# Delaying GpSimd's products of the next half, and moving six weight splits, in a fused linear-attention and two-MLP kernel

## The chip, the cores and the metric

The kernel runs on one core of a Trainium2 chip. The metric is the device time of one execution in microseconds (us), lower is better. The program is written engine by engine: TensorE (matmuls), VectorE, ScalarE, GpSimd and SP (which issues all DMAs) each have a list of instructions that they run in order, and semaphores hold them together.

## The reference

Three stages follow each other: a linear attention with a decaying state, a gated MLP and an ELU MLP. All data is float32.

```python
# r, k, v, w: (B=4, H=8, S=768, D=48); u: (H, D)
for t in range(S):
    cur = einsum('bhd,bhe->bhde', u * kt, vt)
    y[:, :, t] = einsum('bhd,bhde->bhe', rt, state + cur)
    state = wt[..., None] * state + einsum('bhd,bhe->bhde', kt, vt)
x = y.transpose(0, 2, 1, 3).reshape(3072, 384)
x = (sigmoid(x @ w_gate) * (x @ w_val)) @ w_out          # d_ff = 1536
h = x @ w2_in                                            # d_ff = 2048
out = where(h > 0, h, exp(min(h, 0)) - 1) @ w2_out
```

## The kernel before

**Halves.** The sequence is cut into 6 blocks of 128 steps, and each block into two halves of 2 batches: 12 halves q = 0 to 11. Within a half the 16 (batch, head) pairs are worked as G = 8 pairs of heads, in two sub-steps b = 0 and 1 of 4 pairs each. A half is a fixed list of steps (`STAGES`): the transposes Tw, Tr, Tk of w, r and k on TensorE, the levels L1 to L6, the transposes KT of the decayed k, then Y (the output) and S (the new state).

**Levels.** The scores A[s, t] = sum over d of r_t k_s times the decays between s and t are built in levels of block length 1, 2, 4, up to 64. At each level TensorE multiplies (L597, and L603 for the last), VectorE multiplies r by a decay (`next_level_r`, L879, and L883 for the last level), GpSimd multiplies k (`next_level_k`, L513), and VectorE or ScalarE puts the level's scores into A (L922; L711).

**Near entries.** A's diagonal and the entries next to it are not made by matmuls. GpSimd's `term` makes three elementwise products per half: "r'k" (L490, r one step later times k), "rk" (L495) and "u" (L502, two instructions, one per b). VectorE sums them (`sum_after` L888, `sum_own` L892) into `dots`, selects them into `near` (L933, L935) at step L5, and at steps KT copies them into A with a predicated copy (L941), one per b. The semaphore `d_diag` counts these copies. TensorE's Y (L617) of sub-step b waits for it.

**Where the products stand.** At step KT of b = 1 GpSimd first scales the state (L531, two instructions) and then makes the three products of the half q + 1. Nothing of half q holds them; they begin as soon as GpSimd gets there. The sum of "r'k" stands on VectorE's list at step S of the same half, the sum of the others at step Tw of half q + 1.

**Dense work.** Layer 1 of the first MLP is done for sets of tokens as their halves are ready. Its thirds ("g", "v", "o" and a part i = 0 to 2; lines L657 and L666) are interleaved with the attention steps of the next halves in one list, `PROGRAM`, that all engines follow. The first 28 steps are all of half 0 and the first 4 of half 1, and then comes the split of y. float32 operands are cut into a high part (ScalarE, L711) and a low part (VectorE: xl L968, hl L972), and three of the four products are taken. After the attention the second MLP runs alone (L682, L690).

**W1's splits.** The weights of the first MLP lie in 36 pieces (12 column blocks of w_gate, w_val and w_out). Each is loaded by SP (L370, L371, L373) into one of 8 raw places, and split once: ScalarE copies the high part into `WS` and VectorE subtracts it (L993, semaphore `d_wlo`). `SPLIT1` says behind which step of `PROGRAM` each split stands: pieces 0 to 5 behind the steps L5, L6 and KT of half 0, one each, and the others behind each third part of set 0's dense groups. Piece 8 and later ones are loaded into places that an earlier piece leaves, so SP waits for `d_wlo` ahead of them. Pieces 8 to 11 stand on SP's queue just ahead of `move_y(0)` (L380), which brings the rest of half 0's output into place for the dense layer.

Of the kernel before, what the change touches and what calls it, by code (L numbers as in the profile page):

```python
# [13 lines left out]
def build(nc, r, k, v, w, u, w_gate, w_val, w_out, w2_in, w2_out, out):  # L14
# [16 lines left out]
    B, H, S, D = r.shape  # L31
# [8 lines left out]
    U = B // HALF  # L40
# [56 lines left out]
    def count(*use):  # L97

        return PLACE_OF[use] + 1
# [29 lines left out]
    PROGRAM = USES[:LEAD] + [("x", 0)]  # L129
    done = LEAD  # L130
    phase = {}
    for m in range(NS):
        room = len(THIRDS[m]) - (9 if len(SETS[m][1]) == 2 else 14)
        if m + 1 < NS:
# [4 lines left out]
            if m in MORE:  # L139
# [4 lines left out]
                PROGRAM = PROGRAM[:-len(tail)]  # L144
# [8 lines left out]
    assert done == len(USES) and len(set(PROGRAM)) == len(PROGRAM) == len(USES) + NS + sum(len(x) for x in THIRDS + LATE)  # L153

    N1 = 3 * F1
    EARLY = [("a", 0, name, b) for name in ("L5", "L6", "KT") for b in range(U)]
    AHEAD = len(EARLY)

    def splits(step):

        return step in EARLY or (step[:2] == ("d", 0) and step[-1] == 2)


    SPLIT1 = {step: x for x, step in enumerate([step for step in PROGRAM if splits(step)][:N1])}
    SPLIT2 = {("d", NS - 1, "v", j + 1, 2): j for j in range(F1 - 2)}
    assert len(SPLIT1) == N1

    DOWNS = F2 - 1 + B
    STEPS2 = []
# [9 lines left out]
    with ctx:  # L179
# [3 lines left out]
        def sem(name):  # L183
            return ctx.enter_context(nc.semaphore(name))
# [71 lines left out]
        d_w, d_dots, d_near, d_diag = sem("d_w"), sem("d_dots"), sem("d_near"), sem("d_diag")  # L256
# [3 lines left out]
        def wait(eng, s, value):  # L260

            if not (isinstance(value, int) and value <= 0):
                eng.wait_ge(s, value)
# [31 lines left out]
        def level(q, li, b, n=NL):  # L295

            return 2 * n * q + 2 * li + b + 1
# [159 lines left out]
        def _(pool):  # L457
# [50 lines left out]
            def next_level_k(q, li, b):  # L508
                L = 2 ** li
                pool.wait_ge(d_w, NL * q + max(li, 1))  # L510
                Kb = blocks(K[:, b * PR:(b + 1) * PR], L)
                Wb = decay(li)[:, b * PR:(b + 1) * PR].rearrange("q g (i two) -> q g i two", two=2).unsqueeze(4)
                gp.tensor_tensor(Kb[:, :, :, 0, :], Kb[:, :, :, 0, :],  # L513
                                 Wb[:, :, :, 1].to_broadcast([P, PR, P // (2 * L), L]), ALU.mult).then_inc(p_k, 1)

            def attention(q, name, b):
                hf = q % HALF
                if name == "Tk":
                    pool.wait_ge(a_evac, EVAC * q + 4 + b + 1)
                    next_level_k(q, 0, b)  # L520
                elif name[0] == "L":
                    li = int(name[1:])
                    pool.wait_ge(s_att, count("a", q, name, b))
                    pool.wait_ge(p_k, level(q, li - 1, b))
                    next_level_k(q, li, b)
                elif name == "KT" and b == 1:
                    wait(pool, d_s, 2 * q)

                    for e in range(2):
                        rows = slice(e * HP, (e + 1) * HP)  # L530
                        gp.tensor_tensor(SW[rows], ST[rows, hf, :, e, :], decay(NL)[rows].to_broadcast([HP, G, D]),  # L531
                                         ALU.mult).then_inc(p_sw, 1)
                        pool.wait_ge(p_sw, 2 * q + e + 1)
                    if q + 1 < NQ:
                        for part in ("r'k", "rk", "u"):
                            term(q + 1, part)
                if q == 0 and (name, b) in FIRST_TERMS:
                    term(q, FIRST_TERMS[name, b])
# [170 lines left out]
        def _(act):  # L709
            def copy(o, i):  # L710
                return nc.scalar.activation(o, i, ACT.Copy)  # L711
# [86 lines left out]
            def split_w1(x):  # L798
                act.wait_ge(w1_loaded[x], 64 if x % 3 < 2 else 16)
                copy(w1_piece(x, 0), w1_raw(x)).then_inc(a_whi, 1)  # L800
# [43 lines left out]
            for step in PROGRAM:  # L844
                if step[0] == "a":
                    attention(*step[1:])
                elif step[0] == "x":
                    split_y(step[1])
                else:
                    layer1(*step[1:])  # L850
                if step in SPLIT1:
                    split_w1(SPLIT1[step])
                if step in SPLIT2:
                    split_w2(SPLIT2[step])
                if step == ("d", NS - 1, "v", F1 - 1, 2):
                    split_x(0)
# [8 lines left out]
        def _(dve):  # L865
# [125 lines left out]
            def split_w1(x):  # L991
                dve.wait_ge(a_whi, x + 1)
                tt(w1_piece(x, 1), w1_raw(x), f32(w1_piece(x, 0)), ALU.subtract).then_inc(d_wlo, 1)  # L993
# [36 lines left out]
            for step in PROGRAM:  # L1030
                if step[0] == "a":
                    attention(*step[1:])
                elif step[0] == "x":
                    split_y(step[1])
                else:
                    layer1(*step[1:])
                if step in SPLIT1:
                    split_w1(SPLIT1[step])
                if step in SPLIT2:
                    split_w2(SPLIT2[step])  # L1040
                if step == ("d", NS - 1, "v", F1 - 1, 2):
                    split_x(0)
# [26 lines left out]
```

## Time and profile before

| | |
|---|---|
| median of 3 runs | 1128.24 us (1127.53 to 1129.59) |
| profiled execution | 1124.52 us |
| its span | 1122.8 us |
| TensorE matmul busy | 1062.5 us (95%) |
| weight load busy (beside it) | 921.1 us (82%) |
| VectorE busy | 663.4 us (59%) |
| ScalarE busy | 482.6 us (43%) |
| GpSimd busy | 268.2 us (24%) |
| mean granted TensorE clock | 0.977 |

Times in a timeline are microseconds from the start of the span. An instruction's duration includes time in which it is held by a shared resource. A number in brackets behind a row is how long the engine sat idle ahead of it, and what released it. PE is TensorE, DVE is VectorE, ACT ScalarE, POOL GpSimd, and SPq the queue of DMA issues. A granted clock of 1.00 is 2.4 GHz, 0.50 is 1.2 GHz.

### The profile page before, as it was taken

What the parts mean: (1) busy time and instruction counts of PE and PEld (TensorE: products, weight loads), DVE (VectorE), ACT (ScalarE), POOL (GpSimd) and SP (SyncE); (2) the same over time, 40 slices, a digit from 0 to 9 for tenths busy, and PEclk for the clock granted to TensorE, in tenths of its full rate; (3) what the DMA queues carried; (4) which work ended last, traced back from release to release, by engine and by line L of the source; (5) the groups of instructions that cost most, each with busy time, mean ns of one, the idle gap of its engine ahead of it and who ended that gap; (6) DMA issues with size and microseconds to landing.
All of it is one profiled execution on the core that took longest, in us unless ns stands there. A gap on an engine that the chain in (4) does not pass through costs nothing.

```text
span 1122.8 us, 19998 instructions
## 1 busy us (share of the span) xinstructions
PE 1062.5 (95%) x8124; PEld 921.1 (82%) x8124; DVE 663.4 (59%) x914; ACT 482.6 (43%) x895; POOL 268.2 (24%) x258
## 2 busy tenths in 40 slices
PE   4677789999999999999999999999999999999998
PEld 4576778878787888888787888799899999999998
DVE  6878687787948785876678433353434333343433
ACT  2535433534343344334343333464445454454543
POOL 8424162444615351624253100000000000000000
PEclk7699999999999999999999999999999999999999
DMA  7573504041213404050500051120101010010000
GB/s 142 81 134 86 96 2 68 20 65 31 39 46 51 67 2 81 17 68 5 92 5 1 5 155 57 46 82 1 57 2 57 1 43 14 1 57 1 29 1 29
DMA packets 146651, 51.44 MB, mean 46 GB/s; under 512 B 116352, under 2 KB 144256, under 8 KB 146560
## 3 DMA queue, kind: packets, MB, share of 16 engines
q1 hardware_dynamic: 146560, 50.16, 22.4%
q8 instruction: 65, 1.06, 0.4%
q14 instruction: 26, 0.21, 0.1%
HBM read 39.52 MB, written 9.44 MB: 44 GB/s over the span
## 4 chain that ended last, share of the span: by engine, by line
PE 85%; DVE 8%; issue 2%; ACT 2%; SPq 1%; DMA 1%; POOL 0%; DVEq 0%; POOLq 0%; ACTq 0%
PE ps L657 26%; PE ps L690 18%; PE ps L682 17%; PE ps L666 11%; PE ps L597 5%; PE ps L582 3%; PE ps L617 2%; PE ps L623 2%; DVE RKW L879 1%; DVE A L941 1%; DVE A L922 1%; DVE RKW L883 1%; DVE WS L993 1%; PE ps L603 1%; PE ps L631 1%
## 5 line engine op out<-in xcount | busy, mean ns | idle before, releaser
L657 PE MATMUL ps<-xh,WS 128*128 128x512 f32 (+1 forms) x1008 | 255.0, 372 | 19.5 <-DVE xl L968 8.0
L711 ACT ACTIVATE hh<-work 128x512 fp32r<-128x512 f32 (+1 forms) x180 | 108.6, 603 | 297.0 <-DVE work L983 215.0
L657 PEld LDWEIGHTS ps<-xh,WS 128*128 128x128 f32 x1008 | 173.1, 192 | 48.7 <-DVE WS L993 7.7
L690 PE MATMUL ps<-WS,hh 128*128 128x384 f32 x768 | 195.6, 336 | 0.6 <-DVE hl L972 0.6
L972 DVE TENSOR_TENSOR hl<-work,hh 128x512 fp32r<-128x512 f32 (+1 forms) x180 | 130.8, 727 | 96.7 <-ACT hh L711 96.2
L666 PE MATMUL ps<-hh,WS 128*128 128x512 f32 (+1 forms) x504 | 160.7, 373 | 7.1 <-DVE hl L972 7.0
L513 POOL TENSOR_TENSOR RKW<-RKW,WL 128x256 f32<-128x256 f32 x144 | 124.2, 881 | 165.7 <-PE ps L597 141.0
L1010 DVE SCALAR_TENSOR_TENSOR work<-work,ps 128x512 f32<-128x512 f32 x96 | 66.0, 687 | 165.4 <-ACT work L827 165.4
L682 PE MATMUL ps<-xh,WS 128*128 128x512 f32 x576 | 161.5, 392 | 0.0
L690 PEld LDWEIGHTS ps<-WS,hh 128*128 128x128 f32 x768 | 139.8, 188 | 8.1 <-DVE hl L972 1.1
L657 PE MATMUL ps<-xl,WS 128*128 128x512 f32 (+1 forms) x504 | 133.0, 373 | 0.0
L690 PE MATMUL ps<-WS,hl 128*128 128x384 f32 x384 | 128.8, 335 | 0.0
L682 PEld LDWEIGHTS ps<-xh,WS 128*128 128x128 f32 x576 | 106.9, 188 | 17.0
L666 PEld LDWEIGHTS ps<-hh,WS 128*128 128x128 f32 x504 | 93.0, 190 | 25.6 <-DVE hl L972 10.8
L879 DVE TENSOR_TENSOR RKW<-RKW,WL 128x512 f32<-128x512 f32 x120 | 97.3, 840 | 19.0 <-PE ps L597 18.5
L825 ACT ACTIVATE work<-ps 128x512 f32<-128x512 f32 x96 | 57.2, 596 | 109.1 <-PE ps L682 109.1
L657 PEld LDWEIGHTS ps<-xl,WS 128*128 128x128 f32 x504 | 86.7, 192 | 13.8
L597 PEld LDWEIGHTS ps<-RKW 128*64 128x64 f32 x1920 | 67.2, 147 | 30.1 <-DVE RKW L879 18.7
L983 DVE TENSOR_TENSOR work<-work,ps 128x512 f32<-128x512 f32 (+1 forms) x84 | 51.1, 608 | 68.3 <-PE ps L657 57.1
L666 PE MATMUL ps<-hl,WS 128*128 128x512 f32 (+1 forms) x252 | 91.0, 361 | 0.0
L785 ACT ACTIVATE work<-ps 128x512 f32<-128x512 f32 (+1 forms) x84 | 45.0, 536 | 99.8 <-PE ps L657 98.7
L597 PE MATMUL ps<-RKW 128*64 128x64 f32 x1920 | 76.5, 235 | 11.8 <-POOL RKW L513 5.9
(70 smaller groups left out, 1280.6 us busy)
## 6 DMA issues: line engine op xcount, KB each, us to landing
nat<-in_w_dram SPq DMA_DIRECT2D x24, 192.0 KB, 3.6
nat<-in_r_dram SPq DMA_DIRECT2D x24, 192.0 KB, 4.9
nat<-in_k_dram SPq DMA_DIRECT2D x24, 192.0 KB, 5.3
V<-in_v_dram SPq DMA_DIRECT2D x24, 192.0 KB, 4.9
x_scratch<-work SPq DMA_DIRECT2D x12, 384.0 KB, 3.3
nat<-x_scratch SPq DMA_DIRECT2D x6, 768.0 KB, 6.0
out_dram<-A SPq DMA_DIRECT2D x5, 768.0 KB, 4.3
RKW<-in_moe_w_in_dram SPq DMA_DIRECT2D x16, 192.0 KB, 2.4
```

The source lines that it names most:

```text
L513: gp.tensor_tensor(Kb[:, :, :, 0, :], Kb[:, :, :, 0, :], Wb[:, :, :, 1].to_broadcast([P, PR, P // (2 * L), L]), ALU.mult).then_inc(p_k, 1)
L597: last = mm(bank[own, g * C:(g + 1) * C].rearrange("p (e i l) -> p e i l", e=2, l=L), K[:, g, own], Rb[:, :, :, 1, :], start=True, stop=True)
L657: last = mm(ps[:, VAL if val else GATE, t], gate_w(a, val, j, c), xp[b][:, c, t], start=(i == 0 and c == 0), stop=(i == 2 and c == KC - 1))
L666: last = mm(ps[:, ACC + i, t], down_w(a, j, i), hp[b][:, j % 2, t], start=(j == 0 and at == 0), stop=(j == F1 - 1 and at == 2))
L682: last = mm(ps[:, UP2 + j % 4, :], up2_w(a, j, c), xp[b][:, c, :], start=(i == 0 and c == 0), stop=(i == 2 and c == KC - 1))
L690: last = mm(ps[:, ACC2 + b, 0:HD], hp[ap][:, j % 2, b * P:(b + 1) * P], down2_w(wp, j), start=(j == 0 and i == 0), stop=(j == F2 - 1 and i ...
L711: return nc.scalar.activation(o, i, ACT.Copy)
L825: nc.scalar.activation(sig, ps[:, UP2 + j % 4, :], ACT.Relu, scale=-1.0).then_inc(a_relu, 1)
L879: last = tt(Rb, Rb, Wb.unsqueeze(1).unsqueeze(3).to_broadcast([P, 2, n, L]), ALU.mult)
L972: tt(hl[:, j % 2, t], h[:, t], f32(hh[:, j % 2, t]), ALU.subtract).then_inc(d_lo, 1)
L983: tt(h[:, t], sig[:, t], ps[:, VAL, t], ALU.mult).then_inc(d_h, 1)
L1010: nc.vector.scalar_tensor_tensor(h, sig, -1.0, ps[:, UP2 + j % 4, :], ALU.add, ALU.max).then_inc(d_elu, 1)
```

## The change

Two edits. GpSimd waits, ahead of the products for half q + 1, until both near copies of half q are done (`d_diag` at 2(q + 1)); this is so in the halves 0 to 10. And the six splits of W1 that stood one each behind L5, L6 and KT of half 0 stand elsewhere: four behind KT of b = 1, one behind S of b = 1 and one behind Tw of b = 1 of half 1. `SPLIT1` holds a range of pieces for each step instead of one piece; the order of the pieces is the same, and so are all the later places.

```diff
-    EARLY = [("a", 0, name, b) for name in ("L5", "L6", "KT") for b in range(U)]
-    AHEAD = len(EARLY)
-
-    def splits(step):
-
-        return step in EARLY or (step[:2] == ("d", 0) and step[-1] == 2)
-
-
-    SPLIT1 = {step: x for x, step in enumerate([step for step in PROGRAM if splits(step)][:N1])}
+
+    EARLY = {("a", 0, "KT", 1): 4, ("a", 0, "S", 1): 1, ("a", 1, "Tw", 1): 1}
+    AHEAD = sum(EARLY.values())
+
+    SPLIT1 = {}
+    for step in PROGRAM:
+        n = EARLY.get(step, int(step[:2] == ("d", 0) and step[-1] == 2))
+        at = sum(len(x) for x in SPLIT1.values())
+        if n and at < N1:
+            SPLIT1[step] = range(at, min(at + n, N1))
+    assert sum(len(x) for x in SPLIT1.values()) == N1
...
                     if q + 1 < NQ:
+
+                        pool.wait_ge(d_diag, 2 * (q + 1))
                         for part in ("r'k", "rk", "u"):
                             term(q + 1, part)
...
-                if step in SPLIT1:
-                    split_w1(SPLIT1[step])
+                for x in SPLIT1.get(step, ()):
+                    split_w1(x)
```

The last piece stands twice, on ScalarE's list and on VectorE's.

VectorE's list in half 0, from behind the selection of the near entries to the sum into the state. The WS rows are W1's splits, the RKW row of 128 partitions is r at level 5, those of 64 are level 6, A is the near copy and ST the state. Before:

```order
L993 TENSOR_TENSOR WS<-work,WS 128x384
L879 TENSOR_TENSOR RKW<-RKW,WL 128x2x8x32
L993 TENSOR_TENSOR WS<-work,WS 128x384
L883 TENSOR_TENSOR RKW<-RKW,WL 64x4x64 x2
L993 TENSOR_TENSOR WS<-work,WS 128x384
L883 TENSOR_TENSOR RKW<-RKW,WL 64x4x64 x2
L993 TENSOR_TENSOR WS<-work,WS 128x384
L941 COPY_PREDICATED A<-masks,near 128x1024
L993 TENSOR_TENSOR WS<-work,WS 128x384
L941 COPY_PREDICATED A<-masks,near 128x1024
L993 TENSOR_TENSOR WS<-work,WS 128x384
L951 TENSOR_TENSOR ST<-SW,ps 48x8x48 x2
```

The same place after the change, where the same lines have numbers 3 to 5 higher, on to the sixth split (dots are the sums for half 1, WL and RKW<-RKW its first decays):

```order
L884 TENSOR_TENSOR RKW<-RKW,WL 128x2x8x32
L888 TENSOR_TENSOR RKW<-RKW,WL 64x4x64 x4
L946 COPY_PREDICATED A<-masks,near 128x1024 x2
L998 TENSOR_TENSOR WS<-work,WS 128x384 x4
L956 TENSOR_TENSOR ST<-SW,ps 48x8x48 x2
L893 TENSOR_REDUCE dots<-shift 128x16
L998 TENSOR_TENSOR WS<-work,WS 128x384
L961 TENSOR_TENSOR WL<-RKW 128x512
L897 TENSOR_REDUCE dots<-prod 128x16
L998 TENSOR_TENSOR WS<-work,WS 128x384
```

Four splits that stood ahead of the first near copy and one that stood between the copies are gone from there; four stand in a row behind the second copy, and two behind the state's sum. ScalarE's list moves in the same way.

GpSimd's list from the state's products of half 0 to the first product of half 1's level 0, with what each instruction waits for. Before:

```order
L531 TENSOR_TENSOR SW<-ST,WL 64x384
L531 TENSOR_TENSOR SW<-ST,WL 64x384 [waits p_sw]
L490 TENSOR_TENSOR shift<-shift,nat 128x768 [waits shift_loaded,k_loaded,p_sw]
L495 TENSOR_TENSOR prod<-nat 128x768 [waits d_shift,k_loaded,r_loaded]
L502 TENSOR_TENSOR prod<-prod,ub 128x384 [waits p_diag]
L502 TENSOR_TENSOR prod<-prod,ub 128x384
L513 TENSOR_TENSOR RKW<-RKW 128x256 [waits d_w,a_evac] x2
```

After the change:

```order
L534 TENSOR_TENSOR SW<-ST,WL 64x384
L534 TENSOR_TENSOR SW<-ST,WL 64x384 [waits p_sw]
L493 TENSOR_TENSOR shift<-shift,nat 128x768 [waits k_loaded,shift_loaded,d_diag,p_sw]
L498 TENSOR_TENSOR prod<-nat 128x768 [waits d_shift,k_loaded,r_loaded]
L505 TENSOR_TENSOR prod<-prod,ub 128x384 [waits p_diag]
L505 TENSOR_TENSOR prod<-prod,ub 128x384
L516 TENSOR_TENSOR RKW<-RKW 128x256 [waits d_w,a_evac] x2
```

The order is the same; the "r'k" product (shift) waits for `d_diag` as well. Ten more halves have the same piece.

## Rows read from the trace of the kernel before

**Rows 1.** The page: TensorE's busy time; its granted clock in 40 slices.

```profile
PE 1062.5 (95%) x8124; PEld 921.1 (82%) x8124; DVE 663.4 (59%) x914; ACT 482.6 (43%) x895; POOL 268.2 (24%) x258
...
PEclk7699999999999999999999999999999999999999
```

**Rows 2.** Stretches: us, PE, PEld, DVE, ACT, POOL busy, clock, DMA, GB/s.

```profile
100.00:110.00 10.00, 3.26 (x24) 2.82 (x23) 9.58 (x9) 3.81 (x9) 8.23 (x7) 0.91 0.17 50
110.00:120.00 10.00, 10.00 (x124) 9.81 (x124) 5.13 (x9) 5.11 (x14) 0.00 (x0) 0.74 0.22 61
...
330.00:640.00 310.00, 309.67 (x2847) 252.70 (x2846) 229.34 (x296) 121.86 (x236) 124.59 (x116) 1.00 0.25 38
```

**Rows 3.** TensorE's waits: us in total, times, longest.

```profile
PE ps L617 <- DVE A L941: 9.6, 6, 4.7
...
PE ps L657 <- DVE WS L993: 7.3, 2, 6.1
```

**Rows 4.** VectorE, half 1: start, us, line, operation, count, [idle before, releaser].

```profile
102.50 6.25 DVE L883 TENSOR_TENSOR RKW<-RKW,WL 64x256 f32<-64x256 f32 x4
...
111.85 2.50 DVE L941 COPY_PREDICATED A<-masks,near 128x1024 f32<-128x1024 int32 x2
```

**Rows 5.** VectorE by line: ns min/median/max, first and last start.

```profile
L883 DVE TENSOR_TENSOR RKW<-RKW,WL x48: 408/833/2032, 32.8 to 621.8; 64x256 f32<-64x256 f32 x48
L993 DVE TENSOR_TENSOR WS<-work,WS x34: 536/558/2157, 30.8 to 122.8; 128x384 fp32r<-128x384 f32 x34
L941 DVE COPY_PREDICATED A<-masks,near x24: 1291/2858/2971, 37.0 to 624.7; 128x1024 f32<-128x1024 int32 x24
L951 DVE TENSOR_TENSOR ST<-SW,ps x24: 545/552/559, 46.9 to 633.6; 48x384 f32<-48x384 f32 x24
```

**Rows 6.** GpSimd's timeline, half 1.

```profile
102.24 2.01 POOL L490 TENSOR_TENSOR shift<-shift,nat 128x768 f32<-128x768 f32 x1
```

**Rows 7.** VectorE's timeline, half 0.

```profile
36.95 2.90 DVE L941 COPY_PREDICATED A<-masks,near 128x1024 f32<-128x1024 int32 x1
39.74 2.16 DVE L993 TENSOR_TENSOR WS<-work,WS 128x384 fp32r<-128x384 f32 x1
...
46.85 1.14 DVE L951 TENSOR_TENSOR ST<-SW,ps 48x384 f32<-48x384 f32 x2 [1.69 <-PE ps L631]
```

**Rows 8.** GpSimd's timeline, half 0.

```profile
34.05 2.11 POOL L531 TENSOR_TENSOR SW<-ST,WL 64x384 f32<-64x384 f32 x2
...
38.65 2.83 POOL L495 TENSOR_TENSOR prod<-nat 128x768 f32<-128x768 f32 x1
```

**Rows 9.** ScalarE's timeline, half 0.

```profile
33.18 1.20 ACT L711 ACTIVATE A<-ps 64x512 f32<-64x512 f32 x2 [0.32 <-PE ps L603]
```

**Rows 10.** TensorE's timeline, half 0 and the first dense matmul.

```profile
39.99 1.95 PE L617 MATMUL ps<-A,V 128*48 128x128 f32 x16 [4.74 <-DVE A L941]
...
45.83 0.92 PE L631 MATMUL ps<-V,RKW 128*48 128x48 f32 x32
...
53.58 0.89 PE L657 MATMUL ps<-xh,WS 128*128 128x256 f32 x3 [4.38 <-DVE xl L968]
```

**Rows 11.** SP's timeline, half 0.

```profile
46.75 3.77 SPq L380 DMA_DIRECT2D xs<-y  x6
```

**Rows 12.** TensorE's timeline, half 1 and behind it.

```profile
109.39 1.01 PE L657 MATMUL ps<-xh,WS 128*128 128x256 f32 x3 [6.10 <-DVE WS L993]
...
115.45 1.08 PE L617 MATMUL ps<-A,V 128*48 128x128 f32 x16
...
130.23 0.69 PE L597 MATMUL ps<-RKW 128*64 128x64 f32 x16 [1.53 <-POOL RKW L513]
```

**Rows 13.** VectorE's timeline, half 2.

```profile
161.73 5.28 DVE L941 COPY_PREDICATED A<-masks,near 128x1024 f32<-128x1024 int32 x2
```

**Rows 14.** TensorE's timeline, half 2.

```profile
164.35 1.08 PE L617 MATMUL ps<-A,V 128*48 128x128 f32 x16 [2.14 <-DVE A L941]
...
167.16 1.08 PE L617 MATMUL ps<-A,V 128*48 128x128 f32 x16 [0.85 <-DVE A L941]
```

More of the change, by code:

```diff
@@ L155, in build @@
     N1 = 3 * F1
-    EARLY = [("a", 0, name, b) for name in ("L5", "L6", "KT") for b in range(U)]
-    AHEAD = len(EARLY)
-    def splits(step):
-        return step in EARLY or (step[:2] == ("d", 0) and step[-1] == 2)
-    SPLIT1 = {step: x for x, step in enumerate([step for step in PROGRAM if splits(step)][:N1])}
+    EARLY = {("a", 0, "KT", 1): 4, ("a", 0, "S", 1): 1, ("a", 1, "Tw", 1): 1}
[7 more added lines that the diff above has]
+    assert sum(len(x) for x in SPLIT1.values()) == N1
     SPLIT2 = {("d", NS - 1, "v", j + 1, 2): j for j in range(F1 - 2)}
-    assert len(SPLIT1) == N1
     DOWNS = F2 - 1 + B
@@ L1036, in _ @@
                     layer1(*step[1:])
-                if step in SPLIT1:
-                    split_w1(SPLIT1[step])
+                for x in SPLIT1.get(step, ()):
+                    split_w1(x)
                 if step in SPLIT2:
```

## The prediction

> **What bounds the kernel now.** I read the page's engine shares first: TensorE is busy 95% of the span, and its granted clock is full but for the first slices [rows 1]. The table by stretches then says where the missing 5% lie: from 330 to 640 us TensorE is busy 309.67 of 310 us, while from 100 to 110 us it is busy 3.26 of 10 and from 110 to 120 us its clock is 0.74 [rows 2]. So a change of order can only pay ahead of about 200 us, and what it takes off TensorE's waits there is not hidden later, since behind it TensorE simply runs back to back. The waits of TensorE name, among those that end with VectorE, 9.6 us for the near entries (L941) and 7.3 us for W1's splits (L993), of which one is 6.1 us [rows 3].
>
> What makes VectorE late is seen by laying its rows beside GpSimd's. In half 1 four L883 multiplies took 6.25 us together [rows 4], while the fastest of its kind took 0.408 us [rows 5]; GpSimd's products for the next half began at 102.24 [rows 6], beside the first of them. In half 0 a split that began at 39.74 took 2.16 us and ended at 41.90 [rows 7], just behind the product that ended at 41.48 (38.65 + 2.83) [rows 8]. The fastest split took 0.536 [rows 5]. I read this as: a VectorE instruction with two SBUF inputs waits until the GpSimd instruction beside it is done, and then GpSimd waits for it; they alternate. Not every VectorE instruction does: the state's sum L951, with one input in PSUM, stays at 545 to 559 ns in all its 24 places [rows 5].
>
> **The change, part by part.** Nothing is added or removed in arithmetic or DMA; TensorE's and SP's instruction lists stay as they are, and one wait is new on GpSimd in each of 11 halves.
>
> *Half 0, the splits.* Four splits leave VectorE's list ahead of the first near copy, and a fifth from between the copies. The first copy starts at 36.95 now [rows 7]. Without the splits it is ready as soon as ScalarE has put the last scores into A. Those two copies start at 33.18 and take 1.20 [rows 9]; they wait for the level-6 product, which itself comes some 0.4 us earlier without the split between its steps. So the first near copy can start near 34.0, 3 us earlier. Beside it still run the two state products, 2.11 us together [rows 8], which the change doesn't move behind the copies. I take one of them (about 1 us) as held against each copy: a copy is 1.29 alone [rows 5], so they end near 35.9 and 38.05 rather than at 39.85 (36.95 + 2.90). TensorE's Y starts at 35.9 instead of 39.99; from there to the end of the state's product it takes 6.76 us now (45.83 + 0.92 = 46.75 [rows 10]), which I leave as it is, so that product would end near 42.6: 4.1 us won on TensorE.
>
> Most of that I give back. Behind the copies stand four splits, and on GpSimd the four product instructions begin at the same moment. The first split runs free (38.05 to 38.6), the other three wait for one product each: a product of 768 columns takes 2.0 us [rows 6], and of the four the last two have half as many, so 2.0, 2.0, 1.0 and 1.0. That is 38.6 + 2.0 + 0.5 + 2.0 + 0.5 + 1.0 + 0.5 = 45.1. Only then can VectorE add the state, at 46.85 now [rows 7]: 1.75 us earlier, not 4.1. The fifth and sixth split then stand between that sum and the low part of x, about 1.0 us more (two of 0.54 less some overlap). Left: 0.8 us. SP agrees: the loads of W1 ahead of y's moves wait for those splits, the last at about 45.1, and one issue of some 0.4 us follows, so y's moves start near 45.5 instead of 46.75 [rows 11], 1.2 us earlier. The first dense matmul, at 53.58 now [rows 10], comes about **1.0 us** earlier. Bounds: -1.0 (each of the four splits held as long as the one of 2.16, so VectorE is free at 38.05 + 8.6 = 46.7 and the two later splits follow) and 3.1 (no split held: 4.1 less 1.0).
>
> *Half 1, the wait.* The products now start behind the second near copy, so the four L883 run alone: 4 x 0.41 = 1.7 us instead of 6.25, 4.5 us less. TensorE waits 6.10 us at 109.39 for the split right behind them [rows 12]; 1.6 us of it stay. The clock adds to this: after the 6.10 us the three matmuls took 1.01 us, and the stretch 110 to 120 has a mean clock of 0.74 [rows 2], so about half of it ran at 1.2 GHz, whereas after a wait of 1.53 us at 130.23 sixteen small matmuls took 0.69, their time at full clock [rows 12]. So the 6.06 us from 109.39 to Y's start at 115.45 should run at full speed. VectorE limits that: from the end of the four L883 (108.75) to the start of its near copies (111.85 [rows 4]) it takes 3.1 us, and the first copy 1.29 more, so Y can start at 104.2 + 4.4 = 108.6 instead of 115.45, 6.85 us earlier. Given back behind it: the products now lie over two splits and two low parts, of which I expect two or three held, 1.3 us in all. **5.5 us** net. Bounds: 4.0 (the bare 4.5 less a held split) and 6.85.
>
> *Half 2.* The two near copies take 5.28 us together [rows 13]; alone 2 x 1.29 = 2.6, and TensorE waits 2.14 us for the first and 0.85 for the second [rows 14]. Of the 3.0 us I take 2.1, since the second copy already lets Y run on, less 0.6 for the sums behind it, which now meet the last product: **1.5 us**; bounds 0 and 3.0. *Half 3:* of the 9.6 us for near entries 4.74, 2.14 and 0.85 have been counted [rows 10, 14]; of the other 1.9 I take **1.0**; bounds 0 and 1.9. *Halves 4 to 10:* TensorE is back to back [rows 2], so copies that are 1.5 us shorter each bring nothing: **0**. What hides this is TensorE's own queue of dense work; if that cover were gone, it would be 2 x 1.5 us a half. Behind the new wait on GpSimd's own list stands the next half's level-0 product, which needs K's transposes; in half 0 the products would be done near 46, and those transposes follow the first dense matmuls at 53.58 [rows 10], so nobody waits for the products there.
>
> Sum: 1.0 + 5.5 + 1.5 + 1.0 = 9.0 us. The profiled execution took 1124.52 (its span of 1122.8 and 1.7 around it), 3.7 under the median of the three runs, 1128.24. So 1115.5 for an execution like the profiled one, and on the median's scale 1128.24 - 9.0 = **1119.2 us**.
>
> **A rule against the trace.** The row first: L951 stays at 545 to 559 ns in all its places, L883 goes from 408 to 2032 [rows 5]. The Trainium skill (GPSIMD Engine Reference, Key points) says that GpSimd shares its SBUF interfaces with VectorE and names as contending the instructions with two SBUF inputs and those in a 2-port mode. By that rule W1's splits are just the kind to suffer where the change puts them, which speaks against that half of it; it is why the sum has 1.0 and not 3.2 us for half 0. If instead every VectorE instruction were held, the state's sum and the two reductions behind it would be late as well, and half 0 would come out near 0.
>
> **The rivals.** *A: only half 1 pays.* The splits behind the copies cancel half 0, and in halves 2 and 3 the products hold the low parts of h, so that what the near copies win is lost a few us later. For it: one instruction beside a product can grow from 0.54 to 2.16 us [rows 5, 7]. Against: the contention as a whole isn't more than before, and the near copies are the longest VectorE instructions in it. It gives 4.0 to 5.5 us: 1123.5. *B: more than the sum.* The splits aren't held and the low parts find gaps between products: 3.1 + 6.85 + 3.0 + 1.9 = 14.85 us, 1113.4. *C: the wait moves to W1's loads.* SP's loads of W1 feed the splits through half 1; if at 104 us the next piece weren't there, TensorE would wait for DMA instead of VectorE, and with 1.0 us from half 0 and little else the gain would be under 2 us: 1127. For it: each load waits for a split four before it. Against: the 6.10 us are put down to VectorE's split, not to a load [rows 12]. *D: slower.* From half 4 on the four product instructions fall on h's low parts instead of on the near copies. Each can hold one of them 2.0 - 0.4 = 1.6 us (a product of 2.01 [rows 6] less the instruction's own time); if two in each of 7 halves hit a low part for which TensorE has no work left, that is 7 x 2 x 1.6 = 22 us, less 9.0: 1141. It decides from 9.0 / 7 = 1.3 us a half. For it: TensorE has no idle time left there [rows 2], so anything late shows. Against: the same products run in the same halves now beside the same kind of instruction, and TensorE loses 0.33 us in 310. *That the change doesn't do what it says* can't be: the wait stands on GpSimd's list in front of each first product.
>
> **How the numbers follow.** The forecast (7 to 12 us) 0.62; A 0.20; B 0.10; C 0.05; D 0.03. About 0.2% (2.3 us) is what a measurement of this kernel can tell from no change. Forecast, A and B are faster by more than that, 0.92; C is the same, 0.05; D slower, 0.03. The low end takes in the bounds of half 1 and 2 towards B, 1114.0; the high end takes in A with half 1 at its lower bound (4.0), 1124.2.
>
> **What would show it.** Right: near 102 to 104 us four L883 of about 0.42 us; the 6.10 us wait down to 1.5 to 2 and the clock at 1.00 in the ten us behind it; all near copies but those of half 0 at about 1.3 us; splits of 1.0 to 2.4 us behind the near copies of half 0; the first dense matmul at 52 to 53. Wrong: TensorE waits of over 0.5 us from half 4 on for low parts of h (D), a wait of ScalarE for a W1 load near 103 us (C), or the first dense matmul before 51 (B).

## The result and the profile after

| | before | changed |
|---|---|---|
| median of the comparison | 1127.88 us (1125.36 to 1129.59) | 1111.33 us (1110.79 to 1113.07) |
| profiled execution | 1124.52 us | 1110.90 us |
| its span | 1122.8 us | 1109.2 us |
| TensorE busy | 95% | 96% |

The changed kernel is faster: the ratio is 0.9871, with a 95% interval of 0.9845 to 0.9896. That is 16.5 us between the medians and 13.6 us between the two traces. Two later comparisons of the same two kernels gave 0.9905 (0.9877 to 0.9933) and 0.9909 (0.9883 to 0.9934), 10.0 and 11.4 us; over all times on record the medians are 1125.6 (55 times of the kernel before) and 1113.4 (16 of the changed one), 12.2 us apart. The forecast was 1119.2, a gain of 9.0, with a range of 1114.0 to 1124.2; 1111.33 lies below it.

The page of the changed kernel, to be laid beside [rows 1]:

```profile
span 1109.2 us, 20008 instructions
...
PE 1062.6 (96%) x8124; PEld 921.6 (83%) x8124; DVE 630.6 (57%) x914; ACT 482.4 (43%) x895; POOL 249.1 (22%) x258
...
PEclk7699899999999999999999999999999999999999
```

TensorE's waits, as in [rows 3] (us in total, times, longest); line numbers are 3 to 5 higher than before:

```profile
PE ps L662 <- DVE xl L973: 7.6, 3, 5.3
...
PE ps L671 <- DVE hl L977: 5.2, 11, 1.6
...
PE ps L622 <- DVE A L946: 3.0, 4, 1.1
PE ps L662 <- DVE WS L998: 1.6, 1, 1.6
```

The waits for near entries went from 9.6 to 3.0 us and those for W1's splits from 7.3 to 1.6. The wait for the low part of x is nearly as long as before (8.0 us then).

VectorE in half 0, against [rows 7] (start, us, operation, count; the first row starts with the two near copies, the second is the four splits, the third the fourth of them alone, the last the state's sum):

```profile
33.84 3.64 DVE L946 COPY_PREDICATED A<-masks,near 128x1024 f32<-128x1024 int32 x2
37.37 6.01 DVE L998 TENSOR_TENSOR WS<-work,WS 128x384 fp32r<-128x384 f32 x4
...
42.03 1.36 DVE L998 TENSOR_TENSOR WS<-work,WS 128x384 fp32r<-128x384 f32 x1
43.42 1.14 DVE L956 TENSOR_TENSOR ST<-SW,ps 48x384 f32<-48x384 f32 x2
```

GpSimd beside it, against [rows 8]:

```profile
33.47 2.82 POOL L534 TENSOR_TENSOR SW<-ST,WL 64x384 f32<-64x384 f32 x2
37.61 1.98 POOL L493 TENSOR_TENSOR shift<-shift,nat 128x768 f32<-128x768 f32 x1 [1.31 <-DVE A L946]
39.55 2.15 POOL L498 TENSOR_TENSOR prod<-nat 128x768 f32<-128x768 f32 x1
41.77 2.47 POOL L505 TENSOR_TENSOR prod<-prod,ub 128x384 f32<-128x384 f32 x2
```

The first copy starts 3.1 us earlier. The four splits take 6.01 us; alone they would take some 2.1. The fourth ends at 43.39 and the state's sum follows at once.

SP's moves of y, against [rows 11], and TensorE in half 0, against [rows 10]:

```profile
44.38 3.77 SPq L383 DMA_DIRECT2D xs<-y  x6
```

```profile
35.79 1.95 PE L622 MATMUL ps<-A,V 128*48 128x128 f32 x16 [1.11 <-DVE A L946]
...
51.09 0.98 PE L662 MATMUL ps<-xh,WS 128*128 128x256 f32 x3 [5.33 <-DVE xl L973]
```

Half 1, against [rows 4] and [rows 12]. VectorE:

```profile
100.86 1.73 DVE L888 TENSOR_TENSOR RKW<-RKW,WL 64x256 f32<-64x256 f32 x4
...
105.69 2.52 DVE L946 COPY_PREDICATED A<-masks,near 128x1024 f32<-128x1024 int32 x2
```

TensorE:

```profile
103.23 0.62 PE L662 MATMUL ps<-xh,WS 128*128 128x256 f32 x3 [1.58 <-DVE WS L998]
...
107.15 1.08 PE L622 MATMUL ps<-A,V 128*48 128x128 f32 x16 [0.38 <-DVE A L946]
...
130.71 0.62 PE L662 MATMUL ps<-xh,WS 128*128 128x256 f32 x3 [1.59 <-DVE xl L973]
```

The four L883 (L888 now) take 1.73 us instead of 6.25, the 6.10 us wait is 1.58, and Y starts at 107.15 instead of 115.45. Stretches of the changed kernel, against [rows 2]; the last three columns are the granted clock, the DMA share and GB/s:

```profile
100.00:110.00 10.00, 8.04 (x94) 7.63 (x96) 8.12 (x15) 5.86 (x15) 2.18 (x2) 1.00 0.35 98
110.00:120.00 10.00, 9.32 (x114) 9.06 (x111) 7.41 (x12) 5.59 (x14) 4.44 (x4) 1.00 0.05 12
120.00:130.00 10.00, 7.59 (x59) 6.75 (x57) 9.16 (x16) 3.96 (x11) 3.21 (x4) 0.66 1.24 163
130.00:140.00 10.00, 7.73 (x105) 7.12 (x106) 8.17 (x13) 1.40 (x5) 4.47 (x4) 1.00 0.21 55
...
330.00:640.00 310.00, 309.51 (x2787) 252.41 (x2786) 207.19 (x286) 122.92 (x237) 108.45 (x111) 1.00 0.22 37
```

The clock is full from 100 to 120 us, as the forecast had it, but it is 0.66 from 120 to 130, where it was 1.00 in the trace of before, and 1.00 from 130 to 140.

Half 2, against [rows 13] and [rows 14]; first VectorE's near copies, then TensorE:

```profile
152.02 2.49 DVE L946 COPY_PREDICATED A<-masks,near 128x1024 f32<-128x1024 int32 x2
```

```profile
153.46 1.08 PE L622 MATMUL ps<-A,V 128*48 128x128 f32 x16 [0.97 <-DVE A L946]
```

### Where the time went, by stretches that can be compared

The starts of four kinds of row cut each trace into pieces: VectorE's selection of the near entries in half 0 (L933), the first dense matmul, and the state's sums (L951) of halves 1, 2, 3 and 11. Each column is the time from the piece's first row to its last, in us. The first column is the start of the selection itself. The last eight rows are the experiments told in the next section.

| trace | selection at | to first dense | to sum 1 | to sum 2 | to sum 3 | to sum 11 |
|---|---|---|---|---|---|---|
| before | 30.01 | 23.57 | 66.40 | 49.96 | 40.54 | 422.56 |
| before, again | 31.62 | 25.52 | 66.14 | 50.85 | 40.10 | 422.59 |
| changed | 29.91 | 21.18 | 60.58 | 46.32 | 39.03 | 422.40 |
| changed, again | 30.11 | 21.23 | 58.98 | 49.34 | 39.56 | 422.53 |
| changed, third | 30.06 | 21.20 | 60.46 | 46.18 | 38.93 | 422.53 |
| *experiments:* wait alone | 31.70 | 22.06 | 59.59 | 46.30 | 39.02 | 422.55 |
| splits alone | 31.66 | 22.65 | 65.73 | 51.07 | 40.08 | 422.56 |
| splits, wait in half 1 | 31.54 | 22.65 | 59.96 | 51.14 | 40.10 | 422.37 |
| splits, waits in halves 0 to 3 | 31.66 | 21.18 | 59.48 | 49.42 | 39.53 | 422.57 |
| short products in half 0 | 30.02 | 19.46 | 59.19 | 49.04 | 39.51 | 422.63 |
| moves first | 31.81 | 19.12 | 60.57 | 47.99 | 39.13 | 422.42 |
| moves first, again | 29.99 | 19.66 | 60.33 | 48.02 | 39.28 | 422.59 |
| fillers | 30.07 | 22.30 | 59.59 | 48.99 | 39.49 | 422.65 |

Between the first two traces, before and changed, the pieces differ by 0.1, 2.4, 5.8, 3.6, 1.5 and 0.2 us, which is the 13.6.

### The profile page after: what moved, and what is told of

It reads as the page before. It is cut to its first block, busy times and chain, and to the rows that moved or that the text cites. A ratio compares the mean times of both kernels' runs of the same rounds, so it can differ in the third digit from the quotient of the medians.

```text
span 1109.2 us, 20008 instructions
## 1 busy us (share of the span) xinstructions
PE 1062.6 (96%) x8124; PEld 921.6 (83%) x8124; DVE 630.6 (57%) x914; ACT 482.4 (43%) x895; POOL 249.1 (22%) x258
## 4 chain that ended last, share of the span: by engine, by line
PE 85%; DVE 8%; issue 2%; ACT 2%; SPq 1%; DMA 1%; POOL 0%; DVEq 0%; POOLq 0%; ACTq 0%
PE ps L662 25%; PE ps L695 18%; PE ps L687 17%; PE ps L671 11%; PE ps L602 5%; PE ps L587 3%; PE ps L622 2%; PE ps L628 2%; DVE RKW L884 2%; DVE WS L998 1%; DVE A L927 1%; PE ps L608 1%; DVE hl L977 1%; PE ps L636 1%; DVE work L988 1%
## 5 line engine op out<-in xcount | busy, mean ns | idle before, releaser
L662 PE MATMUL ps<-xh,WS 128*128 128x512 f32 (+1 forms) x1008 | 254.0, 371 | 13.6 <-DVE xl L973 7.6
L977 DVE TENSOR_TENSOR hl<-work,hh 128x512 fp32r<-128x512 f32 (+1 forms) x180 | 128.1, 712 | 96.7 <-ACT hh L716 96.2
```

Of the source, the lines that this page charges most:

```text
L662: last = mm(ps[:, VAL if val else GATE, t], gate_w(a, val, j, c), xp[b][:, c, t], start=(i == 0 and c == 0), stop=(i == 2 and c == KC - 1))
L977: tt(hl[:, j % 2, t], h[:, t], f32(hh[:, j % 2, t]), ALU.subtract).then_inc(d_lo, 1)
```

## The experiments

Four variants take the change apart. My theory at this point: the gains add up by place; the wait frees the near copies and L883 of the products in each half, the splits only touch half 0, and part of what the forecast missed is the place in which TensorE's clock falls. The rival: the later halves, or the two edits together, hold it.

### The wait alone

```diff
 (the kernel before)
                     if q + 1 < NQ:
+                        pool.wait_ge(d_diag, 2 * (q + 1))
                         for part in ("r'k", "rk", "u"):
```

> The kernel before with GpSimd's new wait in all 11 halves, the splits where they stood. Theory (places add up: the wait makes the near copies and L883 free of the products in every half, the splits only touch half 0): the near copies of half 0 take 1.3 us each, the first dense matmul comes at 51.5 to 52.5 (53.58 before, 51.09 with both edits), and halves 1 to 3 give the same as with both edits, so 1111 to 1113 us, a span of 1109 to 1111. Rival (the two edits need each other: with the splits in place the half 0 chain stays late): the first dense matmul stays at 53.5 and the time is 1113 to 1115. Second rival (much of the gain in halves 1 and 2 is a lucky clock phase of one trace): the time is 1116 or more.

Measured: 1113.56 us, ratio 0.989 (0.9848 to 0.9933). The near copies of half 0, VectorE:

```profile
38.65 1.30 DVE L942 COPY_PREDICATED A<-masks,near 128x1024 f32<-128x1024 int32 x1
...
40.30 1.31 DVE L942 COPY_PREDICATED A<-masks,near 128x1024 f32<-128x1024 int32 x1
```

They take 1.30 and 1.31 us with the products gone. In the trace of before the first took 2.90 [rows 7] and the second

```profile
41.83 2.10 DVE L941 COPY_PREDICATED A<-masks,near 128x1024 f32<-128x1024 int32 x1
```

The same trace of this variant shows what a product takes while VectorE does nothing, from 42.05 to 47.02 (GpSimd):

```profile
43.67 1.82 POOL L495 TENSOR_TENSOR prod<-nat 128x768 f32<-128x768 f32 x1
```

From the selection to the first dense matmul it takes 22.06 us, 1.5 less than before. The first dense matmul stood at 53.76, outside the expected 51.5 to 52.5, but the selection itself came 1.7 us later in this trace, ahead of anything that the edit touches. By the letter, 53.76 and 1113.56 are what the first rival said (53.5, and 1113 to 1115). Measured from the selection the dense matmul does come earlier, and with 1113.56 against 1126.55 the wait by itself is worth most of the change.

### The splits alone

```diff
 (the changed kernel)
-                        pool.wait_ge(d_diag, 2 * (q + 1))
```

> The changed kernel without the wait. Theory: half 0 gains (first dense matmul at 51 to 52), half 1 keeps four L883 of together 6 us and TensorE's wait of about 6 us behind them, so the gain over the kernel before is only 1 to 2.5 us: 1125 to 1127. Rival (the splits carry the part of the gain that the forecast missed, 4 to 7 us): 1121 to 1124.

Measured: 1123.67 us, ratio 0.9967 (0.9947 to 0.9987), 2.9 us under its comparison's 1126.55; that is more than the theory's 1 to 2.5 and less than the rival's 4 to 7, though the time itself lies in the rival's 1121 to 1124. Half 1 is as before; VectorE and TensorE:

```profile
103.45 6.25 DVE L887 TENSOR_TENSOR RKW<-RKW,WL 64x256 f32<-64x256 f32 x4
```

```profile
110.35 1.01 PE L661 MATMUL ps<-xh,WS 128*128 128x256 f32 x3 [6.11 <-DVE WS L997]
```

To the first dense matmul the splits give 23.57 - 22.65 = 0.9 us, the wait 1.5, and both together 23.57 - 21.18 = 2.4. They add up against this one trace of before. Against its second trace (25.52, see below) they are 2.9, 3.5 and 4.3, so that they add up in general isn't shown.

### The wait in half 1 alone, and in halves 0 to 3 alone

```diff
 (the changed kernel; the second variant has q < 4 in place of q == 1)
+                        if q == 1:
-                        pool.wait_ge(d_diag, 2 * (q + 1))
+                            pool.wait_ge(d_diag, 2 * (q + 1))
```

> The changed kernel with the wait in half 1 alone. Theory: half 1 alone gives 6.4 us of TensorE time, half 0 1.6, and half 2 gives back nothing but keeps its near copies of 5.3 us: the time is 5 us above the changed kernel, 1115 to 1117, less if the matmuls at 131 us run at the high clock anyway. Rival (halves 2 and 3 gain nothing of their own, all is carried from half 1): within 1 us of the changed kernel.

Measured: 1118.93 us, ratio 0.9915 (0.9881 to 0.9949), above the 1115 to 1117 expected. The stretch to sum 1 is 59.96 us against 65.73 without any wait: 5.8 us from half 1 alone. Half 2 has its long wait back, TensorE:

```profile
159.70 1.08 PE L623 MATMUL ps<-A,V 128*48 128x128 f32 x16 [2.13 <-DVE A L947]
```

> The changed kernel with the wait in halves 0 to 3 alone. Theory: from half 4 on TensorE is back to back with or without the wait, so the time is the changed kernel's within 0.5 us, though the near copies of halves 4 to 10 go back to 2.4 to 5.8 us. Rival (the later halves hold part of the gain that the medians show over the traces, 16.5 against 13.6 us): 2 to 3 us slower than the changed kernel.

Measured: 1114.97 us, ratio 0.9875 (0.9841 to 0.9908). That is 3.6 us above the changed kernel's first median, as the rival had it, and 0.5 to 0.8 above its later ones; the pieces decide. Its copies from half 4 on are long again (VectorE):

```profile
246.40 5.81 DVE L947 COPY_PREDICATED A<-masks,near 128x1024 f32<-128x1024 int32 x2
```

and yet the stretch from sum 3 to sum 11 is 422.57 us, against 422.40 to 422.53 in the three traces of the changed kernel and 422.56 before. The waits in halves 4 to 10 are worth nothing that shows. This trace is 4.1 us longer than the changed kernel's first one, though, and 3.1 of it lie between sums 1 and 2, where the two have the same instructions. The stretches around it say what differs:

```profile
120.00:130.00 10.00, 5.68 (x63) 4.82 (x63) 9.19 (x15) 4.66 (x12) 3.29 (x4) 1.00 1.18 149
130.00:140.00 10.00, 8.43 (x89) 7.89 (x90) 5.47 (x10) 0.80 (x2) 2.70 (x3) 0.66 0.31 69
```

```profile
131.57 1.01 PE L663 MATMUL ps<-xh,WS 128*128 128x256 f32 x3 [2.94 <-DVE xl L974]
```

Here the clock is full from 120 to 130 and 0.66 from 130 to 140; the first three matmuls behind the wait for x's low part take 1.01 us, against 0.62 at 130.71 in the changed kernel's trace. That row stands 19.2 us behind sum 1 here and 19.0 in the changed kernel's trace, and from it to sum 2 it is 30.2 us here and 27.3 there. So behind that wait TensorE is the bound, and ahead of it it isn't.

### The changed kernel again

> The changed kernel once more, with nothing edited. Theory (what the forecast missed is in part TensorE's clock, which falls to half speed in one of two places: at about 120 us, where TensorE waits anyway, or at about 131 us, where it is the bound; the four earlier variants had the one or the other with the same instructions there): the trace is either like the first one (state sums of halves 1 and 2 apart by 46.3 us) or like the kernel with waits in halves 0 to 3 (49.4 us), and single times spread over 1110 to 1115 us. Rival (the waits in halves 4 to 10 made the difference of 4 us between those two traces): 46.3 us again, and every time within 1110 to 1112.

Measured: 1114.44 us (1113.09 to 1119.32). To sum 2 it took 49.34 us, 3.0 more than in the first trace of the very same program, and the clock is at half speed in most of the first ten us behind the wait:

```profile
120.00:130.00 10.00, 4.83 (x55) 4.19 (x56) 8.89 (x14) 2.70 (x8) 3.04 (x4) 0.96 1.34 189
130.00:140.00 10.00, 9.47 (x100) 8.72 (x99) 6.00 (x9) 1.18 (x3) 4.46 (x4) 0.70 0.07 24
```

The theory of the clock's place holds, and the rival falls. The clock also makes a difference ahead of sum 1: to there this trace took 58.98 us, 1.6 less than the first, whose clock is 0.83 from 80 to 90 us, where this one's is 1.00. From the selection to sum 2 the two are only 1.5 us apart.

The single times spread wider than the 1110 to 1115 expected, and this trace shows a second source. Two stretches of the second MLP; the number in brackets behind TensorE's busy time counts the matmuls that ran in 60 us, first in the changed kernel's first trace, then in this one:

```profile
820.00:880.00 60.00, 60.00 (x305) 54.40 (x303) 22.89 (x34) 29.02 (x48) 0.00 (x0) 1.00 0.08 27
...
940.00:1000.00 60.00, 60.00 (x305) 54.44 (x304) 23.11 (x35) 29.02 (x48) 0.00 (x0) 1.00 0.08 27
```

```profile
820.00:880.00 60.00, 60.00 (x300) 54.27 (x299) 22.89 (x34) 28.72 (x48) 0.00 (x0) 1.00 0.08 27
...
940.00:1000.00 60.00, 60.00 (x302) 54.45 (x301) 22.24 (x33) 29.35 (x49) 0.00 (x0) 1.00 0.08 27
```

TensorE never waits in either, and both show a granted clock of 1.00, but one makes 305 matmuls in 60 us and the other 300 to 302. From sum 11 to the end of the span it is 489.8 us in the first trace and 495.9 here. The loss is even: each matmul starts 1.6% later behind the one ahead of it.

### Short products beside the splits

```diff
 (the changed kernel; likewise for the three other product instructions)
+                one = slice(0, 1 if q == 1 else D)
-                    gp.tensor_tensor(after, after, own, ALU.mult)
+                    gp.tensor_tensor(after[:, :, one], after[:, :, one], own[:, :, one], ALU.mult)
```

> The changed kernel with GpSimd's four product instructions for half 1 cut to one column of 48 (this changes half 1's diagonal terms). Theory (each of three splits behind the near copies waits for one product, and that holds the state's sum and SP's loads): the four splits take about 2 us together instead of 6.0, the state's sum follows the state's product at once, 1.2 us earlier, and the first dense matmul comes 1.2 to 1.8 us earlier against the near copies; the whole 0.5 to 1.5 us. Rival (nothing waits for these splits): the first dense matmul doesn't move against the near copies.

Measured: 1111.19 us (1110.91 to 1111.52), ratio 0.9871 (0.9837 to 0.9906), 3.25 under the changed kernel on the same chip, more than the 0.5 to 1.5 expected. VectorE and SP:

```profile
37.50 2.05 DVE L999 TENSOR_TENSOR WS<-work,WS 128x384 fp32r<-128x384 f32 x4
40.53 1.14 DVE L957 TENSOR_TENSOR ST<-SW,ps 48x384 f32<-48x384 f32 x2 [0.97 <-PE ps L637]
```

```profile
42.75 3.77 SPq L383 DMA_DIRECT2D xs<-y  x6
```

The four splits take 2.05 us instead of 6.01, VectorE now waits for TensorE ahead of the state's sum, and the way from the selection to the first dense matmul is 1.8 us shorter. The state's sum comes 3.0 us earlier against the selection, not 1.2: part of that is the clock, since the first 16 matmuls of Y took 1.08 us here and 1.95 in the changed kernel's trace. The moves of y don't wait for these matmuls' speed but for SP's loads and so for the splits; they start 1.7 us earlier against the selection. So the products do hold the splits, and that is felt, though by less than the 4 us that they cost VectorE: the low part of x then waits for the moves of y, which wait on SP's queue behind W1's loads.

### A better order: moves first

```diff
-    EARLY = {("a", 0, "KT", 1): 4, ("a", 0, "S", 1): 1, ("a", 1, "Tw", 1): 1}
+    EARLY = {("a", 0, "KT", 1): 3, ("x", 0): 3}
...
+            move_y(0)
             load_w1(NR1 + ONCE, 2 * NR1 + ONCE)
-            move_y(0)
```

> A try at a better order: SP moves y of half 0 ahead of W1's pieces 8 to 11, three splits stand behind the near copies and three behind the low part of x instead of four, one and one. Theory (ahead of the first dense matmul VectorE's list and SP's queue are both just full): the state's sum 1.2 us earlier, the moves at about 42.2 instead of 44.4 us, the first dense matmul 2 us earlier, the whole 1 to 2 us faster than the changed kernel, 1109 to 1110.5. Rival (W1's stage behind it is paced by its own chain of splits and loads): the first dense matmul comes earlier and half 1's state sum doesn't, so the time is the changed kernel's within 0.5 us.

Measured: 1110.71 us (1110.53 to 1112.2), ratio 0.987 (0.984 to 0.990). SP, and then TensorE:

```profile
42.22 3.77 SPq L383 DMA_DIRECT2D xs<-y  x6
```

```profile
50.93 0.98 PE L662 MATMUL ps<-xh,WS 128*128 128x256 f32 x3 [3.94 <-DVE xl L973]
```

The way from the selection to the first dense matmul is 19.12 us, 2.1 less than in the changed kernel, and the state's sum comes 1.3 us earlier against the selection, both as expected. That the moves start at the 42.2 forecast is luck: the selection stood 1.9 us later in this trace than in the changed kernel's.

> The order with y's moves ahead of W1's pieces 8 to 11 and three and three splits, again, beside the changed kernel on one chip. Theory (it takes 2 us off the way to the first dense matmul, and part of it arrives): 1 to 2 us faster than the changed kernel. Rival (the 3.7 us between them in the last comparison were the spread of the runs): within 0.5 us of it.

Measured again beside the changed kernel: 1109.76 us (1107.82 to 1111.36), ratio 0.9854 (0.9835 to 0.9873), against 1114.17. It is faster than both kernels in both comparisons, by 3.7 and 4.4 us against the changed one. The traces don't carry this. The first piece is 2.1 and 1.5 us shorter, and to sum 1 it is 79.7 and 80.0 us, against 80.2 to 81.8. But from the selection to sum 11 it is 589.2 and 589.9 us in the two traces of this order, against 589.5, 591.6 and 589.3 in the three of the changed kernel, because the clock at about 131 us takes some 1.7 us back (48.0 between sums 1 and 2, against 46.2 in two of those three). Two of the changed kernel's three traces have the lower matmul rate in the second MLP and neither of this order's has; whether that is chance I can't say. So the order is faster by its times, and why isn't shown.

### Fillers for the clock

```diff
+            FILLERS = {**{("a", 0, f"L{li}", 1): 5 for li in range(1, NL - 1)}, ("a", 0, "KT", 1): 4, ("a", 1, "Tr", 1): 28}
...
+                for _ in range(FILLERS.get(step, 0)):
+                    nc.tensor.transpose(ps[:, ACC, 0:P], ident[:], ident[:])
```

> The changed kernel with 57 extra transposes of the identity on TensorE into a bank nobody reads yet, where TensorE waits in half 0 and ahead of the first dense matmul. Theory of the clock: the granted clock is 1.00 from 15 to 60 us instead of 0.5 in most of it, the level matmuls of half 0 take 1.1 us instead of 2.2 and the first dense ones 0.5 instead of 0.98, the first dense matmul comes 1 to 3 us earlier and the time falls by 1 to 4 us. Rival (half 0 is bound by VectorE and GpSimd, its matmuls only ride along, or the extra work is itself in the way): no gain, or up to 2 us slower.

Measured: 1113.99 us, ratio 0.9893 (0.9863 to 0.9924); the changed kernel beside it 1114.44. TensorE, the last group of fillers and the first dense matmul:

```profile
45.86 3.22 PE L710 MATMUL ps<-ident 128*128 128x128 f32 x28
52.37 0.98 PE L662 MATMUL ps<-xh,WS 128*128 128x256 f32 x3 [3.29 <-DVE xl L976]
```

The clock was higher, though not full as expected: 0.88 from 20 to 30 us and 0.84 from 30 to 40, against 0.50 in both in the changed kernel's first trace. Yet the selection came no earlier (30.07 against 29.91), so the levels up to there aren't bound by TensorE's clock. Behind it the fillers were themselves in the way: the last level's matmuls, which follow one at 30.04 in the changed kernel, started at 31.05 here, and the near copies at 34.73 against 33.84. The first dense matmul was later too, and after the 3.29 us behind the last filler it ran at 0.98, the low speed: these fillers didn't keep the clock up for it. The rival holds.

### The kernel before again, and the changed kernel a third time

> The kernel before once more, with nothing edited, to have a second trace of it. Theory of the clock: the places in which the granted clock is at half speed ahead of 200 us differ from the first trace's, and the state sums of halves 1 and 2 lie 50 to 51 us apart; the whole is within 1123 to 1129 us. Rival (the same program is granted the same clock): the same state sums within 0.3 us.

Measured: 1126.86 us (1123.31 to 1129.26). The way to the first dense matmul was 25.52 us, 2.0 longer than in the first trace, and the sums 1 and 2 lay 50.85 apart instead of 49.96, with a granted clock of 1.00 and 0.66 in the tens of us from 130 and from 140, where the first trace has 0.95 and 0.88. The theory holds, and the rival (the same sums within 0.3 us) falls.

Of the 2.0 us in half 0, 1.5 are one more split that is held. In the first trace GpSimd's first product had to wait for a load, and the fourth split got ahead of it:

```profile
36.48 0.56 DVE L993 TENSOR_TENSOR WS<-work,WS 128x384 fp32r<-128x384 f32 x1
...
36.74 1.95 POOL L490 TENSOR_TENSOR shift<-shift,nat 128x768 f32<-128x768 f32 x1 [0.58 <-DMA shift<-in_r_dram]
```

In this one the load was there in time, and the product began first:

```profile
37.86 1.87 POOL L490 TENSOR_TENSOR shift<-shift,nat 128x768 f32<-128x768 f32 x1
38.09 2.05 DVE L993 TENSOR_TENSOR WS<-work,WS 128x384 fp32r<-128x384 f32 x1
```

The three traces of the changed kernel, in which no split stands there, agree within 0.05 us (21.18 to 21.23). The forecast was built on an execution of 1124.52 us, near the lower end of this kernel's times, which reach from 1123 to 1130 with two of 1133.6 and 1134.2.

> The changed kernel a third time, with nothing edited, beside the kernel before on one chip. If 16.5 us (the first measurement) is the size of the change, about 1110 against 1126; if 10 us (the second), 1114 to 1115 against 1124. By the traces, 13.6 us with the clock's fall at 120 us and 10 to 11 with the fall at 131 us, I expect 11 to 14 us.

Measured: 1114.17 us (1113.04 to 1121.44), 11.4 under the kernel before, inside 11 to 14.

## Why the prediction was wrong

**The direction, the places and the mechanism were right.** TensorE's waits in halves 0 to 3 were the only place for a gain; VectorE's instructions with two SBUF inputs were held by GpSimd's products; and in halves 4 to 10 nothing came, since 422.4 to 422.6 us lie between sums 3 and 11 in every trace. **The size was wrong:** 9.0 us forecast, 13.6 between the traces. The 7.9 us between 1119.2 and the 1111.33 measured are 4.6 us that the sum of the gains lacks and 3.3 us in the step from one execution to a median. The terms that failed are half 2 (1.5 forecast, 3.6 measured: the clock was priced at nothing there), half 0 (1.0 and 2.4: the price of a pair of split and product), and the 3.7 us between execution and median, taken as fixed (0.4 in the changed kernel's measurement).

- **Half 0: 1.0 forecast, 2.4 measured** (23.57 to 21.18; within its bounds). The first near copy came at 33.84, as forecast (34.0). The failed step is the price of a pair behind it. I put a product of 2.0 us and the held split's own 0.5 one behind the other, 2.5 us a pair. But the 2.0 was read beside a L883 that took its turn too [rows 6]: alone a product takes 1.82 us. The held splits ended at 40.0, 42.1 and 43.39, so a pair of one long product costs 2.1 us. Three held splits took 5.5 us (37.9 to 43.39), not 6.5, and the copies ended at 37.47, not 38.05. The size also depends on the trace of before: against its second one (25.52) half 0 gave 4.3 us, more than the upper bound of 3.1.
- **Half 1: 5.5 forecast, 5.8 measured** (66.40 to 60.58; 5.8 again from the wait alone on equal splits, 65.73 to 59.96). These steps held: 1.73 us for the four L883 (1.7), 1.58 of the wait left (1.6), full clock behind it, and Y 8.3 us earlier, of which 1.65 came from half 0 and 6.65 here (6.85). What was to be given back, 1.3 us to held splits and low parts behind Y, wasn't: the state's sum, at 119.98 before and 111.67 now, is 8.3 us earlier as well. In its place 0.8 us were lost ahead of the L883, where the clock is 0.83 from 80 to 90 us and 1.00 in the trace of before. The changed kernel's second trace, with full clock there, has 58.98, a gain of 7.4 and above the bound of 6.85. That 5.8 came so near to 5.5 is in part luck.
- **Half 2: 1.5 forecast, 3.6 measured** (49.96 to 46.32; its bounds were 0 and 3.0). This is the largest miss. The near copies themselves are worth 1.7 us (51.14 with the wait in half 1 alone, 49.42 with it in half 2 too, the clock 0.66 from 130 to 140 us in both), so that part of the term was sound. The other 1.9 us are the place of the clock's fall: 120 to 130 us, where TensorE waits anyway, instead of 130 to 150, where it is the bound. The changed kernel had 46.2, 46.3 and 49.3 us here in three traces. The forecast priced the clock in one place, behind the 6.10 us, and nowhere else.
- **Half 3: 1.0 forecast, 1.5 measured.** Where the clock is full in this piece it takes 40.1 us without the wait (splits alone, the wait in half 1, before again) and 39.0 with it (changed, wait alone), so 1.1 us are the wait's, as forecast. The other 0.4 are the clock, 0.83 from 180 to 190 us in the first trace of before and 1.00 in the changed kernel's.
- **From an execution to a median.** I subtracted the gain from the median and took the 3.7 us between the profiled execution and the median as fixed. They aren't: repeated comparisons give 10.0, 11.4 and 16.5 us for the same pair, and the first happened to hold times of the kernel before from the upper part of its spread and times of the changed one from the lower part. The median of three that I started from, 1128.24, is 2.6 us above the median of all 55 times. 1111.33 lies 2.7 us under the range's low end; the other two medians, 1114.44 and 1114.17, lie inside it, just above its low end.

**The rivals.** B (more than the sum) was the nearest to the first measurement, though not by its mechanism: the splits were held. A, C and D didn't come: no wait moved to W1's loads, and no half from 4 on lost anything. The rule of the Trainium skill that the prediction named (GPSIMD Engine Reference, Key points) held where it mattered: the splits with two SBUF inputs went from 0.54 to 2.18 us beside products, while the state's sum, with one input in PSUM, stays at 546 to 559 ns, with the products still running beside it in half 0 (43.42 against a product until 44.2). The prediction took this contrast from the trace of before, where it hardly showed: only 2 of the 24 state's sums stood beside a GpSimd instruction there. In the changed kernel's trace 8 do, and none of them is longer.

## What to carry to other kernels

An engine with slack can still hold the bound engine through the one between them: ask which of its instructions must run now, and let the others wait until the urgent neighbour is past, here with one semaphore wait. Such a wait is worth what the bound engine stands idle for at that place, and nothing where it has a queue of its own work. A forecast within 1% of a kernel whose clock falls somewhere in it needs the spread of several traces first, since one trace fixes the clock's place by chance.

## What the runs showed of the hardware

- TensorE's granted clock falls to half speed in places that differ between executions of one program, and where it falls decides up to 3 us: the stretch between sums 1 and 2 took 46.2 to 49.3 us in three traces of the changed kernel.
- The levels of half 0 have two forms as well: the near entries' selection starts at 29.9 to 30.1 or at 31.5 to 31.8 us. The granted clock doesn't explain them: from 10 to 20 us it is 0.63 and from 20 to 30 it is 0.50, both in the changed kernel's first trace (29.91) and in that with the wait in half 1 alone (31.54). What does is open.
- At a granted clock of 1.00 and with no wait, TensorE made 305 matmuls in 60 us in one trace of the changed kernel and 300 to 302 in another. From sum 11 to the end it is 489.4 to 489.8 us in eleven of the thirteen traces and 495.9 in two, both of the changed kernel. The profile's busy, clock and DMA columns show no cause.
- VectorE instructions with two SBUF inputs wait for the GpSimd product beside them, and the product waits for its turn in between. Beside splits nearly all of the loss is VectorE's: the four took 6.01 us instead of 2.05, one of them up to 2.18, while the two products of 768 columns beside them took 1.98 and 2.15, against 1.82 alone and 2.83 for the one beside a near copy in [rows 8].
